# Attention output made transposed in 32-column tiles, with the state's increment behind scores times values

## What is computed

```python
f = 1.0 / (1.0 + np.exp(-f_logit))
for t in range(S):
    state = f[:, :, t, :, None] * state + np.einsum('bhd,bhe->bhde', k[:, :, t], v[:, :, t])
    y[:, :, t] = np.einsum('bhd,bhde->bhe', q[:, :, t], state)
x = y.transpose(0, 2, 1, 3).reshape(B * S, H * D)
h = x @ moe_w_in                                      # 384 x 2048
x = (np.maximum(h, 0) + np.log1p(np.exp(-np.abs(h)))) @ moe_w_out
h = x @ moe2_w_in                                     # 384 x 2048
g = np.where(h >= 1, h, np.where(h <= -1, 0, (h + 1) ** 2 / 4))
return g @ moe2_w_out
```

## Time and profile before

| | |
|---|---|
| runs shown | 1793.07 us median of 3 (977.71, 1793.07, 2409.6) |
| profiled execution | 979.63 us, span 977.9 us |
| mean granted PE clock | 0.984 |
| busy: PE, DVE, ACT, POOL | 96%, 55%, 47%, 9% |
| chain that ended last | 88% PE, 5% DVE, 3% ACT |
| loaded or stored by DMA | 46.5 MB, 48 GB/s mean |

### The profile page before, as it was taken

The page is one execution under the profiler, slowest core; times in us unless marked ns, Lnnn a source line. Parts: engine busy times, 40 slices in busy tenths (PEclk is TensorE's granted clock), DMA queues, the critical chain, the costliest instruction groups (busy, mean ns, idle before and its releaser), DMA issues.

```text
span 977.9 us, 13426 instructions
## 1 busy us (share of the span) xinstructions
PE 942.7 (96%) x5048; PEld 808.1 (83%) x5048; DVE 542.0 (55%) x920; ACT 456.4 (47%) x861; POOL 89.8 (9%) x71
## 2 busy tenths in 40 slices
PE   5879999999999999999999999999999999999996
PEld 3779999899888888888888888888888888888885
DVE  5865465655565665555634665555555555555543
ACT  3455666555555656465557863233233332332322
POOL 4331021211111111011100010000000000000000
PEclk9599999999999999999999999999999999999999
DMA  8811123213121121314003311010010010100000
GB/s 193 226 34 33 34 58 66 50 34 65 50 41 33 33 66 33 61 38 130 1 1 114 97 47 35 1 64 1 1 66 1 32 34 1 64 1 1 33 1 35
DMA packets 18806, 46.54 MB, mean 48 GB/s; under 512 B 1968, under 2 KB 6192, under 8 KB 18736
## 3 DMA queue, kind: packets, MB, share of 16 engines
q1 hardware_dynamic: 18736, 45.62, 18.0%
HBM read 36.18 MB, written 9.44 MB: 47 GB/s over the span
## 4 chain that ended last, share of the span: by engine, by line
PE 88%; DVE 5%; ACT 3%; issue 2%; DMA 1%; POOL 0%; SPq 0%; DVEq 0%; ACTq 0%; POOLq 0%
PE h_ps L465 13%; PE y_ps L465 13%; PE y_ps L467 13%; PE y_ps L466 12%; PE h_ps L467 12%; PE h_ps L466 12%; PE a_ps L544 4%; PE a_ps L523 2%; PE a_ps L540 2%; DVE dec L803 2%; PE c_ps L530 1%; DVE g_lo L784 1%; PE c_ps L512 1%; PE b_ps L550 1%; ACT soft L627 1%
## 5 line engine op out<-in xcount | busy, mean ns | idle before, releaser
L784 DVE TENSOR_TENSOR g_lo<-gate,g_hi 128x512 fp32r<-128x512 f32 (+2 forms) x208 | 149.2, 717 | 342.2 <-ACT g_hi L643 342.2
L465 PE MATMUL y_ps<-g_hi,w_hi 128*128 128x512 f32 (+2 forms) x624 | 234.7, 376 | 12.7 <-DVE g_lo L784 8.0
L465 PE MATMUL h_ps<-x_hi,w_hi 128*128 128x512 f32 (+2 forms) x624 | 239.6, 384 | 1.2 <-DVE gate L768 1.2
L467 PE MATMUL y_ps<-g_hi,w_lo 128*128 128x512 f32 (+2 forms) x624 | 233.2, 374 | 0.0
L466 PE MATMUL y_ps<-g_lo,w_hi 128*128 128x512 f32 (+2 forms) x624 | 233.1, 374 | 0.0
L466 PE MATMUL h_ps<-x_lo,w_hi 128*128 128x512 f32 (+2 forms) x624 | 233.1, 374 | 0.0
L467 PE MATMUL h_ps<-x_hi,w_lo 128*128 128x512 f32 (+2 forms) x624 | 232.9, 373 | 0.0
L631 ACT ACTIVATE soft<-h_ps 128x512 f32<-128x512 f32 x96 | 57.4, 598 | 260.0 <-PE h_ps L467 260.0
L465 PEld LDWEIGHTS y_ps<-g_hi,w_hi 128*128 128x128 f32 x624 | 117.6, 188 | 36.1 <-DVE g_lo L784 17.2
L465 PEld LDWEIGHTS h_ps<-x_hi,w_hi 128*128 128x128 f32 x624 | 117.7, 189 | 23.0 <-issue 1.5
L467 PEld LDWEIGHTS h_ps<-x_hi,w_lo 128*128 128x128 f32 x624 | 117.4, 188 | 19.4
(11 more groups left out here) (78 smaller groups left out, 797.9 us busy)
## 6 DMA issues: line engine op xcount, KB each, us to landing
qkf_sb<-qkf SPq DMA_DIRECT2D x48, 288.0 KB, 4.8
w_raw<-w SPq DMA_DIRECT2D x32, 384.0 KB, 5.0
v_sb<-v SPq DMA_DIRECT2D x24, 192.0 KB, 5.1
x_in<-x_mid SPq DMA_DIRECT2D x6, 768.0 KB, 5.9
out<-y_sb SPq DMA_DIRECT2D x6, 768.0 KB, 3.8
x_mid<-y_sb SPq DMA_DIRECT2D x4, 768.0 KB, 4.9
x_mid<-y_sb SPq DMA_DIRECT2D x2, 576.0 KB, 3.4
x_mid<-y_sb SPq DMA_DIRECT2D x1, 384.0 KB, 2.8
```

The lines of the kernel that those rows point to most:

```text
L465: nc.tensor.matmul(out_ap, hi1, hi2, start=start, stop=False, skip_group_check=True)
L467: return nc.tensor.matmul(out_ap, lo1, hi2, start=False, stop=stop, skip_group_check=True)
L784: nc.vector.tensor_tensor(g_lo[:, t % 2, 0:g.n], gate[:, t % 2, 0:g.n], g_hi[:, t % 2, 0:g.n].bitcast(F32), ALU.subtract).then_inc(glo_don ...
```

## The change

Three things are changed, and a few follow from them.

The result of a unit is made with channels on partitions, as the first layer needs it, in `c_ps`: 28 matmuls, each with 32 columns of weights (of the state, or of the values) and 128 moving columns (queries, or scores). Four of them in a row write the four groups of 32 partitions of one block. A head's first 32 channels fill a group of the first two blocks. The last 16 channels of both heads of a pair share a group of the third block, for which the values come with zeros in between: `v` grows from 384 to 640 columns, and the rows of `moe_w_in` are put in the same order on the host. `y_att`, its copy on ACT and the three transposes are gone, and `main` has four pieces in place of five: ACT's copy to `x_hi` stands at s = 2.

The state's increment is made behind that, in `a_ps`, with a semaphore of its own (`kv_done`); the state's two heads are stored interleaved.

The order by hand before the first layer is another, one `keep_warm` matmul at unit 0 is gone, slices 7, 10, 13, 14 and 15 go from POOL to DVE, and `x_in` shares its memory with `qkf_sb`. The next load of a unit waits for `kv_done` too.

```diff
-STAGES = 5
+STAGES = 4
+HALF = 32
@@ first_group
             main(0, 2)
+            main(0, 3)
             prep(2, 3)
             main(1, 1)
...
-            return m in (1, 4, 7, 10, 13, 14, 15, 2 * FT - 2, 2 * FT - 1)
+            return m in (1, 4, 2 * FT - 2, 2 * FT - 1)
@@ PE, main(u, s)
                 if s == 0:
                     pe.wait_ge(k_done, u + 1)
                     if u >= 2:
-                        pe.wait_ge(state_done, before + 1)
+                        pe.wait_ge(xlo_done, before + 1)
...
-                if s == 1 and not new_batch(u):
+                if s == 1:
                     pe.wait_ge(k_tok_done, u + 1)
-                    for p in range(PAIRS):
-                        c = slice(p * 2 * D, (p + 1) * 2 * D)
-                        mm = nc.tensor.matmul(c_ps[0:ROWS, c], k_tok[:, p, :], v_sb[:, j, c],
-                                              start=True, stop=True, skip_group_check=True)
-                if s == 1:
-                    if first:
-                        keep_warm(1)
-                    pe.wait_ge(masked, u + 1)
                     if not first:
                         pe.wait_ge(state_done, u)
-                    for p in range(PAIRS):
-                        c = slice(p * 2 * D, (p + 1) * 2 * D)
-                        nc.tensor.matmul(a_ps[:, c], q[0:ROWS, p, :], state[0:ROWS, p, :],
-                                         start=(p == 0), stop=False, skip_group_check=True)
-                        for a in range(2):
-                            c = slice((2 * p + a) * D, (2 * p + a + 1) * D)
-                            mm = nc.tensor.matmul(a_ps[:, c], scores[:, a, p, :], v_sb[:, j, c],
-                                                  start=False, stop=True, skip_group_check=True)
+                    st = state[0:ROWS].rearrange("p q (e a) -> p q e a", a=2)
+                    for tile in range(KT):
+                        t = slice(tile * P, (tile + 1) * P)
+                        for j in range(4):
+                            pair = 2 * tile + j // 2 if tile < 2 else j
+                            lhs = st[:, pair, 0:HALF, j % 2] if tile < 2 else state[0:ROWS, pair, 2 * HALF:2 * D]
+                            nc.tensor.matmul(c_ps[HALF * j:HALF * (j + 1), t], lhs, q[0:ROWS, pair, :],
+                                             start=(tile == 0), stop=False, skip_group_check=True)
+                    pe.wait_ge(masked, 2 * u + 2)
+                    for tile in range(2):
+                        t = slice(tile * P, (tile + 1) * P)
+                        for j in range(4):
+                            h = 4 * tile + j
+                            nc.tensor.matmul(c_ps[HALF * j:HALF * (j + 1), t], v_sb[:, slot, h * D:h * D + HALF],
+                                             scores[:, h % 2, h // 2, :], start=False, stop=True, skip_group_check=True)
+                    t = slice(2 * P, 3 * P)
+                    for a in range(2):
+                        for j in range(4):
+                            h = 2 * j + a
+                            mm = nc.tensor.matmul(c_ps[HALF * j:HALF * (j + 1), t],
+                                                  v_sb[:, slot, DM + h * HALF:DM + (h + 1) * HALF],
+                                                  scores[:, a, j, :], start=False, stop=True, skip_group_check=True)
                     mm.then_inc(ya_done, 1)
-                if s == 2:
-                    pe.wait_ge(ya_copied, u + 1)
-                    for k in range(KT):
-                        mm = nc.tensor.transpose(b_ps[:, k * P:(k + 1) * P], y_att[:, k * P:(k + 1) * P], ident[:])
-                    mm.then_inc(xt_done, 1)
+                    if not new_batch(u):
+                        for p in range(PAIRS):
+                            c = slice(p * 2 * D, (p + 1) * 2 * D)
+                            mm = nc.tensor.matmul(a_ps[0:ROWS, c], k_tok[:, p, :], v_sb[:, slot, c],
+                                                  start=True, stop=True, skip_group_check=True)
+                        mm.then_inc(kv_done, 1)
@@ ACT, main(u, s)
                 if s == 2:
-                    act.wait_ge(ya_done, u + 1)
-                    nc.scalar.activation(y_att[:], a_ps[:, 0:DM], ACT.Copy).then_inc(ya_copied, 1)
-                if s == 3:
-                    split_x(u, b_ps)
+                    split_x(u, c_ps)
@@ DVE, main(u, s), s == 2
-                    dve.wait_ge(ya_done, u + 1)
+                        dve.wait_ge(kv_done, u - u // CHUNKS + 1)
```

More of the change, by code:

```diff
@@ L277, in first_group @@
             main(1, 2)
+            main(1, 3)
             split_w(5)
@@ L505, in main @@
                 a_ps, b_ps, c_ps = banks(u)
-                q, k = qkf_sb[:, j, 0], qkf_sb[:, j, 1]
+                q, k = qkf_sb[:, slot, 0], qkf_sb[:, slot, 1]
                 if s == 0:
@@ L691, in split_x @@
                 nc.scalar.activation(x_hi[:, g.par, :, c],
-                                     b_ps[:, 0:DM].rearrange("p (k t) -> p k t", k=KT), ACT.Copy).then_inc(xhi_done, 1)
+                                     c_ps[:, 0:DM].rearrange("p (k t) -> p k t", k=KT), ACT.Copy).then_inc(xhi_done, 1)
             def split_x_in(g, k):
-                act.wait_ge(x_in_s, 16 * (g.G - len(LAYER0) + 1 - sum(h.layer == 2 and h.index == 0 and 0 for h in GROUPS)))
+                act.wait_ge(x_in_s, 16 * (g.G - len(LAYER0) + 1))
                 act.wait_ge(h_done, FT * (g.G - 1))
@@ L830, in main @@
                 if s == 2:
-                    dve.wait_ge(ya_done, u + 1)
-                    blocks = [(slice(64 * a, 64 * a + D), slice(a * D, (a + 1) * D)) for a in range(2)]
+                    st = state[:].rearrange("p q (e a) -> p q e a", a=2)
+                    blocks = [(slice(64 * a, 64 * a + D), a) for a in range(2)]
                     if new_batch(u):
+                        dve.wait_ge(ya_done, u + 1)
                         nc.vector.memset(state[:], 0.0).then_inc(state_done, 1)
@@ L835, in main @@
                     else:
-                        for rows, cols in blocks:
-                            inc = c_ps[rows, 0:DM].rearrange("p (a e) -> p a e", a=PAIRS)[:, :, cols]
-                            nc.vector.tensor_tensor(state[rows, :, cols], inc, state[rows, :, cols],
+                        dve.wait_ge(kv_done, u - u // CHUNKS + 1)
+                        for rows, a in blocks:
+                            inc = a_ps[rows, 0:DM].rearrange("p (q a e) -> p q a e", q=PAIRS, a=2)[:, :, a, :]
+                            nc.vector.tensor_tensor(st[rows, :, :, a], inc, st[rows, :, :, a],
@@ L840, in main @@
                                                     ALU.add).then_inc(added, 1)
                         dve.wait_ge(added, ADDED[u] + 2)
-                        for rows, cols in blocks:
+                        for rows, a in blocks:
                             by = inv[rows, j, :, P - 1:P].to_broadcast([D, PAIRS, D])
-                            last = nc.vector.tensor_tensor(state[rows, :, cols], state[rows, :, cols], by, ALU.mult)
+                            last = nc.vector.tensor_tensor(st[rows, :, :, a], st[rows, :, :, a], by, ALU.mult)
@@ L854, in split_x @@
                 c = slice((u - g.unit) * P, (u - g.unit + 1) * P)
-                nc.vector.tensor_tensor(x_lo[:, g.par, :, c], b_ps[:, 0:DM].rearrange("p (k t) -> p k t", k=KT),
+                nc.vector.tensor_tensor(x_lo[:, g.par, :, c], c_ps[:, 0:DM].rearrange("p (k t) -> p k t", k=KT),
                                         x_hi[:, g.par, :, c].bitcast(F32), ALU.subtract).then_inc(xlo_done, 1)
```

113 lines of the change are left out of this document (61 added, 52 removed).

## The result

The changed kernel takes 954.62 us (median of 4 runs, 952.97 to 955.20) against runs of the kernel before at 977.71 and 981.93 us: a ratio of 0.9736, 95% interval 0.9705 to 0.9768. The sum forecast 955.4. The two slow runs of the kernel before (1793 and 2410 us) are not compared: their cause isn't known, and none of the 17 later runs of that kernel, at 976.6 to 982.3 us, was like them.

The account below looks back on a forecast made before the run. PE was taken to bound the kernel inside the layer, with DVE sharing the chain at the start. 979.6 - 21.0 (1.00 us in 21 units) - 3.2 (start) = 955.4 us, 2.5% less; eight in ten from 947 to 982.

Parts of the forecast that it names:

- the piece: PE's work at s = 1 of each unit, result and increment: 2.82 us forecast, 0.66 less than 3.48.
- The start: Stretch before the layer's steady part, four terms: 3.2 us gained, between -3 (a loss) and 7.
- (d): Start, second gate: five slices on DVE replace a slow `g_lo`; first gate to PE's restart 10.1 to 11.7 us, taken as even.
- The step of four: Result at s = 1: four matmuls writing four partition groups run together, 14 steps of 0.11 us; chance 0.55, total 955.
- Ways in and out: Around the narrow matmuls at s = 1, PE changes its array's division: 0.20 us in and 0.20 out per unit.
- The transposes: Three per unit on PE behind the result, all gone: 0.34 us saved per unit, 21 units.
- At nothing: Other moves in the layer on ACT, DVE and loads are covered and cost nothing; if covers fail, 4 us at most.
- (a): Start: unit 0's load grows by 128 KB, so its first work comes 0 to 1.0 us later; 0.7 taken.
- (c): Start, chain from unit 1's mask to `x_lo` of unit 2, PE at half clock: done at 45.1 us for 48.3.
- Feeding PE: Rival: PE's instruction feeding, about 0.028 us each, limits s = 1 to 3.0 to 3.8 us; total 968, chance 0.27.
- Two at a time: Rival: only two narrow matmuls run together at s = 1, making it 4.4 us; total 989, chance 0.08.
- The rule on 62 ns per matmul: Skill page's sequencer limit on PE: 56 records would take 3.5 us for 1.57, total about 995.

Follow-up runs that it names:

- experiment 3: Changed kernel with all 28 narrow matmuls writing partitions 0 to 31, so nothing can run together; output is not attention's: 1054.20 us, ratio 1.0749 to the kernel before.
- experiments 1 and 2: Changed kernel with narrow matmuls reordered: 1, one partition group after another, 968.54 us; 2, groups 0 and 1, then 2 and 3, 958.01 us.
- experiment 5: Changed kernel with the increment between state times queries and values times scores, dividing the array four times per unit: 957.08 us, ratio 0.9765 to the kernel before.
- experiment 6: Changed kernel with three 128 x 128 transposes put back on PE at s = 2, their result unread: 960.51 us, ratio 0.9795 to the kernel before.
- Experiment 4: Changed kernel with the increment matmuls ahead of the narrow ones, behind the wait for the mask: 955.52 us, ratio 0.9745 to the kernel before.
- experiment 7: Changed kernel with weight slices 7, 10, 13, 14 and 15 on POOL again: 954.42 us, ratio 0.9734 to the kernel before.

## Why the prediction was right or wrong, by its steps

**In short.** The mechanism was right, and what failed are sizes of terms in the sum. The layer's stretch of 20 units gave 22.3 us for 20.0, because the piece was put at 2.82 us and takes 2.65, less 0.9 us of longer waits; the term furthest off in it is the way in, 0.20 for a measured 0.11. The start gave 2.0 us for 3.2, because term (d), from the first gate to PE's restart, was taken as even with 10.6 us and took 12.5, of which 1.0 us is left at unit 3's keys. With 1.0 as forecast for unit 23 the sum is 25.3 for 24.2. So the errors, 2.3 us one way and 1.2 the other, cancel in part, and that the total is right within 1 us is luck to that extent. The base was chosen rightly: beside the shown median of 1793.07 a time of 955 would be 47% less, and the change is 2.6%; the later runs of the kernel before lie within 3.1 us of the 979.6 that the sum started from.

**The bound.** Right. 22.3 of 25.3 us came from PE's own work in the 20 units, at nearly one to one.

**The step of four.** Right: 14 steps of 0.109 for 14 of 0.112. The scores' pair was the right row to go by, and experiment 3 shows the other end of the bound at its price. Its reason was half right: that separate parts of the array run together. I took it that neighbours in the program do; experiments 1 and 2 show that PE looks for work of a free group further on, by a few records.

**Ways in and out.** The sum had 0.20 and 0.20. The changed kernel shows 0.11 in (in single records the second step stands at 304.52, where 304.41 would be unhindered) and 0.19 out, and experiment 5 shows 0.30 for another pair. The way in was mis-sized by 0.09 us per unit. The row that it was taken from, the scores, has 128 columns of weights behind the change, and here it is 32; that this is the reason is likely, not shown.

**The piece.** 2.65 for 2.82: 0.83 saved for 0.66 forecast; the 0.09 above, 0.04 from the steps, and the rest is spread over the joints.

**The transposes.** Right: 0.33 for 0.34. But their worth is less than 21 x 0.33, as experiment 6 shows, since some of the time turns into waits for `g_lo`.

**At nothing.** Nearly: PE waits 0.9 us more behind `g_lo`, within the bound of 4. That is why 0.83 + 0.33 = 1.16 per unit arrive as 1.11. Experiment 4 bears out that the increment's place costs nothing that its runs show.

**The start.** 3.2 forecast; 3.0 at `x_lo` of unit 2, and 2.0 at unit 3's keys. (a) ACT's first operation came 0.8 later, for 0.7; but nine traces with the same loads have it between 8.01 and 9.32, so this trace doesn't resolve the term.

(c) took PE at half clock up to `x_lo` of unit 2. It wasn't, as the windows from 37 to 40 us show (us, busy us and instructions of PE, PEld, DVE, ACT and POOL, then the granted clock), before and after:

```profile
37.00:40.00 3.00, 3.00 (x23) 2.78 (x21) 2.66 (x5) 3.00 (x6) 1.18 (x1) 0.50 0.53 173
```
```profile
37.00:40.00 3.00, 1.86 (x40) 1.43 (x40) 2.92 (x6) 3.00 (x5) 0.00 (x0) 1.00 0.90 315
```

The granted clock is 1.00 from 37 to 43 us, where it was 0.50. So from the end of unit 2's mask to the end of its `x_lo` it took 4.6 us (40.7 to 45.3) for 5.7 forecast. But that mask ended 1.3 us later than forecast, (a) included. On DVE two slices ahead of it took twice their 0.93 each:

```profile
32.71 3.68 DVE L867 TENSOR_TENSOR w_lo<-w_raw,w_hi 128x768 fp32r<-128x768 f32 x2
```

The two nearly cancel, so the 3.0 for 3.2 at `x_lo` of unit 2 is in part luck.

(d) was called even, between 10.1 and 11.7 us from the first gate to `down`; it took 12.5 (49.90 to 62.37), just outside. The last slice waited for its load, and the nine matmuls of `up` ran at half clock (0.32 us apart for 0.17). By unit 3's keys that is 1 us lost against before. The hand-made order, the missing `keep_warm` and the slices were not run apart from each other, but for the slices in experiment 7.

**Rivals.** Feeding PE is no limit at 0.11 us for four matmuls and four loads. These are eight instructions; the prediction's sixteen, and its "four times what any row shows", are twice too many. Its price for this rival came from the right count, 112 instructions in the piece. Two at a time didn't occur, not even where the program asked for it. The rule on 62 ns per matmul (the Trainium skill, "TensorE: Matmul & The Clock Gate", section "Wait — 56ns, not 53.3ns?") doesn't bind here: four matmuls start per 0.109 us, 0.027 each. By the same page, section "Measured speedup vs the span model", three column tiles are 2.38 times as fast as one at 512 moving columns; the trace shows 4.0 times for four (7.22 less 1.15 for ways and increment is 6.07 us for one group, and 1.53 for four), at 128 moving columns.

## What to carry to other kernels

A matmul with few moving columns doesn't get cheaper with them: with 128 columns of weights, records that move 96 and 48 columns start 0.11 us apart alike (with 112 columns of weights 0.10), so it is likely the load of the weights that is paid; no run changed it alone. Turn such a matmul round, so that 32 columns are loaded and the long side moves, and spread the results over the four groups of 32 partitions: 56 records took 1.5 us where 24 took 2.6, and the transposes behind them went as well. The gain is the groups' running together and not the short load: one group alone took 6.1 us. Interleave the groups, but count the changes in how the array is divided, each pair 0.3 to 0.4 us, and put work of one kind together. When PE is the bound and gets faster, look at the start next, where DVE, POOL and the loads set the pace: moving five slices there was worth a quarter of what the change was (6.9 of 25.3 us).

## What the runs showed of the hardware that I had not expected

PE doesn't start matmuls in the order of the program when they go to different column groups: with the groups in line, records of a later loop started 0.3 us ahead of the last of an earlier one (312.72 and 313.04). The order cost 0.73 us per unit. In strict order, with groups overlapping only where they meet, it would need 45 steps for 14.4, an estimate of 3.3 us more. But PE looks only a few records ahead: a free group stayed idle for 0.25 us, until three records of the group before it had started.

Four groups step together every 0.109 us, with four matmuls and four loads, the same step as for one group alone.

`g_lo` on DVE, beside three slices on POOL, ended 0.41 us behind POOL's last in both traces that have the pair (63.42 and 59.80 us), though it had started 5.21 and 2.03 us before its end. The first gate's, with none of these slices beside it, takes 0.56.
